# Expert rows loaded in four column strips and turned by VectorE instead of TensorE, with the expert weights stored to match

## The reference, cut to what matters

```python
logits = x @ w_gate                      # x: 4352 x 512
e_idx = np.argmax(logits, axis=1)
gate_w = probs[np.arange(N), e_idx]      # softmax of the logits
eom = 1.0 / (1.0 + np.exp(-(x @ w_output_gate)))
for e in range(E):                       # E = 8
    mask = e_idx == e
    h = np.maximum(x[mask] @ w1[e], 0.0) # w1[e]: 512 x 1024
    ye = h @ w2[e]                       # w2[e]: 1024 x 512
    out[mask] = gate_w[mask, None] * eom[mask, e, None] * ye
```

## Time and profile before

| | |
|---|---|
| median of three runs | 1226.95 us (1226.36 to 1226.95) |
| the profiled execution: its own time | 1227.15 us |
| the profiled execution: span of the trace | 1225.3 us |
| PE busy | 1189.3 us, 97% of the span |
| DVE busy | 580.4 us, 47% |
| ACT busy | 445.3 us, 36% |
| mean granted TensorE clock | 0.986 of full |
| row loads `xg<-buckets` | 41, 258.0 KB each, median 2.6 us from issue to landing |

### The profile page before, as it was taken

How to read it: one execution, slowest core, us unless ns; L and a number is a source line. 1 busy time by engine, 2 the same in 40 slices (tenths; PEclk the granted TensorE clock), 3 DMA queues, 4 the chain that set the end, 5 groups by cost and what they waited for, 6 DMA issues and landing times.

```text
span 1225.3 us, 20849 instructions
## 1 busy us (share of the span) xinstructions
PE 1189.3 (97%) x6808; PEld 939.2 (77%) x6809; DVE 580.4 (47%) x1100; ACT 445.3 (36%) x741; POOL 84.0 (7%) x96
## 2 busy tenths in 40 slices
PE   7999999999999999999999978999999999999995
PEld 6777777777777777777778866888888888878874
DVE  4564645645547455465554373553532223455221
ACT  3454434443444344443544332341411112344110
POOL 0000100101001000010010110200000000000000
PEclk8999999999999999999999988999999999999998
DMA  9110100001001111010100662514151110541111
GB/s 369 63 36 1 69 36 35 36 35 70 35 14 56 36 47 58 1 70 1 69 36 1 221 207 100 179 43 175 37 179 52 34 51 28 181 163 44 41 36 42
DMA packets 32266, 91.45 MB, mean 75 GB/s; under 512 B 2879, under 2 KB 4031, under 8 KB 29632
## 3 DMA queue, kind: packets, MB, share of 16 engines
q1 hardware_dynamic: 26432, 72.56, 17.0%
q0 software_dynamic: 5760, 17.90, 3.8%
HBM read 65.95 MB, written 25.55 MB: 75 GB/s over the span
## 4 chain that ended last, share of the span: by engine, by line
PE 93%; DVE 3%; ACT 1%; issue 1%; DMA 0%; DVEq 0%; ACTq 0%; POOL 0%; SPq 0%; POOLq 0%
PE y_ps L829 30%; PE h_ps L894 17%; PE y_ps L920 17%; PE h_ps L814 14%; PE y_ps L906 3%; PE a_ps L789 2%; PE h_ps L804 2%; PE a_ps L876 1%; PE a_ps L679 1%; PE a_ps L767 1%; PE a_ps L740 1%; PE b_ps L687 1%; DVE we L462 1%; PE b_ps L679 0%; DMA x_t<-in_x_t 0%
## 5 line engine op out<-in xcount | busy, mean ns | idle before, releaser
L829 PE MATMUL y_ps<-w_out_hi,hid_hi 128*128 128x512 f32 x544 | 220.4, 405 | 0.3 <-DVE w_out_lo L1328 0.3
L829 PE MATMUL y_ps<-w_out_hi,hid_lo 128*128 128x512 f32 x544 | 212.8, 391 | 0.0
L829 PE MATMUL y_ps<-w_out_lo,hid_hi 128*128 128x512 f32 x544 | 212.5, 391 | 0.0
L894 PE MATMUL h_ps<-we,xg_t_hi 128*128 (+1 forms) x608 | 195.5, 403 | 4.6 <-DVE we L462 2.0
L920 PE MATMUL y_ps<-we,act_t_hi 128*128 (+1 forms) x608 | 191.4, 396 | 2.2 <-issue 2.2
L814 PE MATMUL h_ps<-att_hi,mix 128*128 128x512 f32 x512 | 186.6, 408 | 0.0
L1343 DVE SCALAR_TENSOR_TENSOR hid<-hid,h_ps 128x512 f32<-128x512 f32 (+1 forms) x144 | 94.4, 655 | 182.8 <-ACT hid L1038 181.3
L1038 ACT ACTIVATE hid<-h_ps,three 128x512 f32<-128x512 f32 (+1 forms) x144 | 95.5, 663 | 204.2 <-PE h_ps L814 180.8
L829 PEld LDWEIGHTS y_ps<-w_out_hi,hid_hi 128*128 128x128 f32 x544 | 102.1, 188 | 51.2 <-issue 30.4
L894 PEld LDWEIGHTS h_ps<-we,xg_t_hi 128*128 128x128 f32 x608 | 112.2, 189 | 30.6 <-issue 6.2
L920 PEld LDWEIGHTS y_ps<-we,act_t_hi 128*128 128x128 f32 x608 | 111.4, 188 | 24.3 <-issue 2.7
(11 more groups left out here) (227 smaller groups left out, 1341.6 us busy)
## 6 DMA issues: line engine op xcount, KB each, us to landing
raw<-in_w SPq DMA_DIRECT2D x14, 2048.0 KB, 8.8
xg<-buckets SPq DMA_DIRECT2D x41, 258.0 KB, 2.6
xb<-in_x_rows SPq DMA_DIRECT2D x8, 1024.0 KB, 4.8
x_t<-in_x_t SPq DMA_DIRECT2D x7, 1024.0 KB, 5.5
buckets<-pad_row SPq DMA_DIRECT2D x8, 774.0 KB, 8.6
w_in_raw<-in_w_in SPq DMA_DIRECT2D x4, 1024.0 KB, 13.2
raw_out<-in_w_out SPq DMA_DIRECT2D x4, 1024.0 KB, 14.8
x_t_second<-in_x_t SPq DMA_DIRECT2D x1, 1024.0 KB, 19.7
```

The lines of the kernel that those rows point to most:

```text
L829: i = pe.matmul(y_ps[:, t, :], (hid_hi, hid_lo)[hp][:, hid_at(b, j), t * P:(t + 1) * P], w_out_s[wp][:, j, :], start=(j == 0 and m == 0), ...
L894: i = pe.matmul(hid_ps[:, h, :], xg_t[xp][:, slot % 2, k, :], we[:, bass.ds(w_at + (wp * WPART + k * F + h * BANK), BANK)], start=(k == 0 ...
```

## The change

A tile's rows are no longer loaded with one row on each partition. Column quarter j (128 columns) of all 128 rows goes to partitions 32j to 32j+31: partition 32j+t holds rows t, 32+t, 64+t and 96+t, 128 columns each. Four DMAs do this, and a fifth one loads the last four columns (gate factor and token number) of each row to a new tile `gate_s`. DVE then turns the tile by one `transpose`, which swaps partition and column within every 32x32 block, into `xg_raw`. `xg_raw` lies at the same address as `xg_t[LO]`; `rows_lo` subtracts in place. Partition 32j+d, chunk k of the result holds column 128j+32k+d, so w1 is stored in DRAM in that order of its rows, [E, 128, 4, F]; w2 is stored as [E, 128, 8, 512]. Both are then loaded with one contiguous run for each partition. PE's `transpose_rows` is gone.

```
@@ addresses
-    xg = at("xg", 163840, [P, RING, ROW], F32)
+    STRIPS = P // NS
+    xg = at("xg", 163840, [P, RING, STRIPS, P], F32)
+    gate_s = sb("gate_s", [P, RING, ROW - DM])
+    xg_raw = at("xg_raw", late_at + 12288, [P, 2, KD, P], F32)
@@ SP, load_rows
-            sp.dma_start(xg[:, slot, :], buckets[bass.ds(r, P), :]).then_inc(sem(f"xg_loaded{slot}"), 16)
+            tile_rows = buckets[bass.ds(r, P), :]
+            for j in range(STRIPS):
+                sp.dma_start(xg[NS * j:NS * j + NS, slot, :, :],
+                             tile_rows[:, P * j:P * j + P].rearrange("(s t) c -> t s c", t=NS)
+                             ).then_inc(sem(f"xg_loaded{slot}"), 16)
+            sp.dma_start(gate_s[:, slot, :], tile_rows[:, DM:ROW]).then_inc(sem(f"gate_loaded{slot}"), 16)
@@ SP, load_expert (the first loads likewise)
-            sp.dma_start(raw1[:].rearrange("p (k f) -> p k f", k=KD),
-                         w1[bass.ds(e, 1)].rearrange("o (k p) f -> p (o k) f", p=P)).then_inc(sem("raw1_loaded"), 16)
+            sp.dma_start(raw1[:], w1[bass.ds(e, 1)].rearrange("o p k f -> p (o k f)")
+                         ).then_inc(sem("raw1_loaded"), 16)
@@ PE
-        def transpose_rows(t):
-            slot = t.slot
-            wait(pe, f"xg_loaded{slot}", 16 * (t.turn() + 1))
-            wait(pe, "xg_t_ready", t.n)
-            for k in range(KD):
-                i = pe.transpose(a_ps[:, 0, k * P:(k + 1) * P], xg[:, slot, k * P:(k + 1) * P], ident[:])
-            i.then_inc(sem("xg_t_ps"), 1)
...
-            if not t.last:
-                transpose_rows(t.plus(1))
...
-        transpose_rows(Tile(0, 0))
@@ ACT, rows_hi
-            wait(act, "xg_t_ps", t.n + 1)
-            act.activation(xg_t[HI][:, slot % 2, :, :].rearrange("p k t -> p (k t)"), a_ps[:, 0, :], ACT.Copy
+            wait(act, "xg_turned", t.n + 1)
+            wait(act, "hid2_ps", HALVES * (t.n - 1) if not t.first else 0)
+            act.activation(xg_t[HI][:, slot % 2, :, :], xg_raw[:, slot % 2, :, :], ACT.Copy
@@ DVE, rows_lo subtracts from xg_raw in the place of a_ps; new beside it:
+        def turn_rows(t):
+            slot = t.slot
+            wait(dve, f"xg_loaded{slot}", 16 * STRIPS * (t.turn() + 1))
+            if not t.first and not is_b(t.n, 1):
+                wait(dve, "hid2_ps", HALVES * (t.n - 1))
+            dve.transpose(xg_raw[:, slot % 2, :, :].rearrange("p k t -> p (k t)"),
+                          xg[:, slot, :, :].rearrange("p s (k d) -> p k s d", d=NS)).then_inc(sem("xg_turned"), 1)
@@ DVE, start of the experts' part
         dve.tensor_copy(table[:, T_NEXT, MT:MT + 1], second[:]).then_inc(sem("second_ready"), 1)
+        turn_rows(Tile(0, 0))
         split_lo(dve, 1, 0, 0, (0,))
         rows_lo(Tile(0, 0))
...
         dve.sem_inc(sem("table_ready"), 1)
+        turn_rows(Tile(0, 1))
         split_lo(dve, 1, 0, 0, range(1, PIECES), "w2_ready")
@@ DVE, put_out waits for gate_loaded and reads gate_s; at the end of DVE's body(t):
+            if not (isinstance(t.n, int) and t.n + 2 >= MT):
+                turn_rows(t.plus(2))
```

More of the change, by code:

```diff
@@ L45, in emit_kernel @@
     E = w1.shape[0]
-    F = w1.shape[2]
+    F = w1.shape[3]
     SCALE = float(D) ** -0.5
@@ L524, in _ @@
         sp.wait_ge(sem("lt_ps"), B - 1)
-        sp.dma_start(raw1[:].rearrange("p (k f) -> p k f", k=KD),
-                     w1[0].rearrange("(k p) f -> p k f", p=P)).then_inc(sem("raw1_loaded"), 16)
+        sp.dma_start(raw1[:], w1[0].rearrange("p k f -> p (k f)")).then_inc(sem("raw1_loaded"), 16)
         sp.wait_ge(sem("pad_row_ready"), 2)
@@ L539, in _ @@
         sp.wait_ge(sem("h_ps"), KF * (B + 1))
-        sp.dma_start(raw2[:].rearrange("p (j d) -> p j d", j=KE), w2[0].rearrange("(j p) d -> p j d", p=P)
-                     ).then_inc(sem("raw2_loaded"), 16)
+        sp.dma_start(raw2[:], w2[0].rearrange("p j d -> p (j d)")).then_inc(sem("raw2_loaded"), 16)
         def load_rows(t):
@@ L555, in load_expert @@
             wait(sp, "w1_ready", n)
-            sp.dma_start(raw1[:].rearrange("p (k f) -> p k f", k=KD),
-                         w1[bass.ds(e, 1)].rearrange("o (k p) f -> p (o k) f", p=P)).then_inc(sem("raw1_loaded"), 16)
+            sp.dma_start(raw1[:], w1[bass.ds(e, 1)].rearrange("o p k f -> p (o k f)")
+                         ).then_inc(sem("raw1_loaded"), 16)
             wait(sp, "w2_ready", n)
-            sp.dma_start(raw2[:].rearrange("p (j d) -> p j d", j=KE),
-                         w2[bass.ds(e, 1)].rearrange("o (j p) d -> p (o j) d", p=P)).then_inc(sem("raw2_loaded"), 16)
+            sp.dma_start(raw2[:], w2[bass.ds(e, 1)].rearrange("o p j d -> p (o j d)")
+                         ).then_inc(sem("raw2_loaded"), 16)
         sp.wait_ge(sem("rows_stored"), 16 * N_SCATTER)
@@ L583, in all_loaded @@
                 tiles = min(t.n + RING, MT)
-                sp.wait_ge(sem(f"xg_loaded{s}"), 16 * ((tiles - s + RING - 1) // RING))
+                sp.wait_ge(sem(f"xg_loaded{s}"), 16 * STRIPS * ((tiles - s + RING - 1) // RING))
+                sp.wait_ge(sem(f"gate_loaded{s}"), 16 * ((tiles - s + RING - 1) // RING))
         loops(sp, body, all_loaded)
@@ L1397, in rows_lo @@
             wait(dve, "xg_t_hi", t.n + 1)
-            dve.tensor_tensor(xg_t[LO][:, slot % 2, :, :].rearrange("p k t -> p (k t)"), a_ps[:, 0, :],
-                              xg_t[HI][:, slot % 2, :, :].rearrange("p k t -> p (k t)").bitcast(F32), ALU.subtract
+            dve.tensor_tensor(xg_t[LO][:, slot % 2, :, :], xg_raw[:, slot % 2, :, :],
+                              xg_t[HI][:, slot % 2, :, :].bitcast(F32), ALU.subtract
                               ).then_inc(sem("xg_t_ready"), 1)
+        def turn_rows(t):
[5 more added lines that the diff above has]
+                          xg[:, slot, :, :].rearrange("p s (k d) -> p k s d", d=NS)).then_inc(sem("xg_turned"), 1)
         steps = [0]
@@ L1507, in put_out @@
                 wait(dve, f"out_stored{prev.slot}", 16 * (prev.turn() + 1))
-            dve.tensor_copy(out_row[:, slot:slot + 1], xg[:, slot, TOKEN:TOKEN + 1])
-            dve.tensor_scalar(yo[slot % 2][:], y2_ps[:, slot % 2, :], xg[:, slot, GATE:GATE + 1], None, ALU.mult
+            wait(dve, f"gate_loaded{slot}", 16 * (t.turn() + 1))
+            dve.tensor_copy(out_row[:, slot:slot + 1], gate_s[:, slot, TOKEN - DM:TOKEN - DM + 1])
+            dve.tensor_scalar(yo[slot % 2][:], y2_ps[:, slot % 2, :], gate_s[:, slot, 0:1], None, ALU.mult
                               ).then_inc(sem("out_ready"), 1)
@@ L1583 @@
     give("gates", gates.reshape(-1, 128, 4 * E).transpose(1, 0, 2))
-    give("w1", inputs["moe2_w1"])
-    give("w2", inputs["moe2_w2"])
+    give("w1", inputs["moe2_w1"].reshape(E, 4, 4, 32, -1).transpose(0, 1, 3, 2, 4).reshape(E, 128, 4, -1))
+    give("w2", inputs["moe2_w2"].reshape(E, -1, 128, DM).transpose(0, 2, 1, 3))
     n = B * (S + NS)
```

## The result

The changed kernel takes 1209.25 us (median of four runs, 1208.65 to 1210.2), the kernel before beside it 1226.65 us: a ratio of 0.986 with a 95% interval of 0.9843 to 0.9878, 17.4 us less. The profiled execution took 1208.73 us, with a span of 1207.0 us.

What follows compares the result with a forecast made beforehand. PE, busy 97% of the span, was taken to bound the steady tiles with its matmuls, DVE's chain the start; -16.3 + 2.3 - 0.9 = -14.9 us from 1227.15 gave 1212.3, as median 1212.0, range 1208.5 to 1218.5.

Steps and rivals of the forecast that it cites:

- PE's 0.44 us a tile: Steady tiles on PE: removing the four row transposes saves 0.44 us in each of 37 tiles, 16.3 us.
- the low bound of 0.35: Lower price of a tile's four row transposes on PE, from the spacing of their starts: 0.35 us, 13.0 us in all.
- the full duration of 272 ns: Rival for PE's row transposes: each saves its whole 272 ns, 40.3 us in all, giving 1188 us; chance 0.01.
- The junction: PE from `first` to `second`: its sequencer is over 2 us ahead, so closing the gap costs nothing.
- A turn of 0.7 us: DVE's transpose of a tile's rows takes 0.7 us, bounds 0.42 and 2.8, hidden in steady tiles.
- The start, 2.3 us: Start, on DVE's chain: a wait for strips and two turns, 0.9 + 0.7 + 0.7, delay the relu by 2.3 us.
- The term for the strips' wait: Start: DVE waits 0.9 us for tile 0's last strip, issued about 1.1 us after row 0's load, landing in 2.6.
- The stall, 0.9 us: Three-tile expert: PE's 1.98 us wait for w1's split shortens by about 0.9 us; bounds 0 and 1.98.
- The loads: SP's queue: five DMAs a tile for one, 0.33 us each; rows still arrive in time, so nothing is charged.
- The slower rival: Strips land too late for the four-tile loop; landing above 19.6 us takes back all gain; near 1250 us; chance 0.03.
- The sum: Whole kernel: the terms -16.3 + 2.3 - 0.9 give -14.9 us.

Runs made afterwards that it cites:

- e2: The changed kernel with four row transposes a tile put back on PE behind `first`, their result read by nobody: 1226.57 us.
- e3: The changed kernel with every tile turned twice by DVE, the second turn waiting for the first: 1211.58 us.
- e1: The kernel before with only the stored order of w1 and w2 and their loads changed: 1226.93 us, ratio 1.0001.
- e8: As e7, and ACT and DVE read their three table entries at the top of every body but the first: 1204.12 us.
- e5: The changed kernel with 155 small matmuls in the place of 100 before tile 0: 1210.38 us.
- e4: The changed kernel with each strip loaded by two DMAs of 64 columns in the place of one: 1213.23 us.
- e7: The changed kernel with 155 small matmuls for 100 and three pieces of w2's first split moved to the end of DVE's first body: 1206.97 us.
- e11: The changed kernel with the w2 split pieces moved, table entries read early and 130 small matmuls in the place of 100: 1205.43 us.

## Why the prediction was right, and where it was off

**PE's 0.44 us a tile.** Right: 0.46. The forecast took 37 * 0.44 = 16.3; measured are 36 * 0.46 = 16.6 and one more in tile 1, 17.0. The rest is in the w2 matmuls, whose piece on the chain is 5.47 us for 5.49. e2 settles the cause: the same 17.3 us come back when PE does idle transposes. It also settles that the low bound of 0.35 and the full duration of 272 ns were wrong prices.

**The junction.** Right: `second` follows `first` without a gap; the lead of PE's sequencer was enough. Only in the last tiles, behind the hardware loop, did some of the saved time come back, ahead of `first`: the chain has 0.19 and 0.17 us of issue there, for 0.09 and 0.09 before.

**A turn of 0.7 us.** Right: 701 ns, close to the 690 ns of the plain one-pass operation on 128x512 in the earlier trace rows. The Trainium skill (Vector Engine (DVE) Microarchitecture Reference, section 3.8) has the transposing front end sustain one element per cycle and lane; the trace agrees in that the turn takes as long as a plain pass over as many elements. The turn is hidden in the steady part even when doubled (e3).

**The start, 2.3 us.** The mechanism was right; the size was 1.5 in this profile. The term for the strips' wait was 0.9 and measured 0.39: SP took 0.44 us for a strip and not 0.33, but the data of the last strip was there 1.9 us after its issue and not 2.6. The two turns cost 0.64 us each on DVE's chain, and 0.3 us came back because the small operations around them ran that much earlier than before, counted from the last MLP matmuls. Counted so, DVE's relu moved by 1.35 us. e2, whose only edit is PE's idle transposes, has 2.2 us in the place of 1.5 because DVE came to its first turn 0.8 us later, and the kernel before with the weights' order changed (e1) starts 0.5 us later than before with no turn at all. So one profile each does not settle whether 2.3 was too much. The wait itself goes up to 2.30 us (e8) where a code load falls in with the strips, as told at e5.

**The stall, 0.9 us.** Nearly right: 0.74. ACT's split moved 2.35 us after its relu, as the step said, and DVE's was held by its relu and table reads; e8 shows that these reads are what was left of the stall.

**The loads.** The conclusion, nothing charged, was right; its number was not. The step took the longest landing before, 8.1 us, as the bound. Behind two weight loads the four strips took 12.6 us, and e4, with 14.4 and a later issue, shows PE 1.6 us late. The step was right that PE needs the turned rows only one tile later; what it did not work out is how little of that tile is left behind such a load, some 2.3 us. The slower rival asked for over 19.6 us in every tile; it overlooked that a single late tile, behind a weight load, already costs PE time.

**The sum.** 14.9 forecast, 17.4 measured. The terms as measured in the profiles, -17.0 + 1.5 - 0.7, give -16.2; the table without its first line gives -18.42 + 1.85 = -16.6, and the gap of 0.48 us that is gone is most of the rest. The difference between either and 17.4 is within what two medians of four runs are uncertain by (the interval of the ratio is 4.3 us wide). How much of it is the granted clock of tile 1's `first`, 7.24 us here and 8.5 in the profiles of e5, e7 and e8, is open. So the main term was hit closely and for its reason. The measured time lies near the fast end of the range, and of the 2.5 us by which the sum was short no more than about 1.7 can be traced to its terms.

## What to carry to other kernels

When one engine sets the pace, price what leaves it by the spacing of starts on the chain, not by durations, and check that its sequencer runs far enough ahead to close the gap. Moving work to an engine with half of its time free is free only where that engine does not lead: look separately at the start, where it often does. An in-order engine that waits for a DMA holds everything behind it, so the landing that counts is the longest one behind the largest transfer in the same queue. A change in the number of instructions on one engine can also move when code is loaded, so look at the DMA queues at that place before a difference is put down to the clock.

## What the runs showed of the hardware that was not expected

- Four strips of 64 KB, issued right behind two loads of 2 MB on SP, had landed 12.6 us after the first issue (the changed kernel); the same rows in eight DMAs took 14.4 us (e4). With no weight load ahead, the last strip was there 1.9 us after its issue.
- Issuing a strip on 32 partitions took SP about 0.44 us (1.76 for four), a whole-row load on 128 took 0.33.
- Where a code load of 0.02 MB fell among the strips of tile 0 (e5, e7, e8, e11), DVE waited 1.25 to 2.30 us for them, in the other six kernels with five loads 0.39 us or less. In e2, where it came at 728 to 730 us, SP needed 2.77 us to issue four strips at 729.28, for 1.81 in the changed kernel. That one causes the other is not shown.
- A fp32 transpose of 32x32 blocks over 128x512 took VectorE 701 ns (the changed kernel, median of 40).
- The granted clock of PE is not set by the program alone. Between 12 and 25 us, with the same instructions, its mean was 0.74 (before), 0.87 (e1) or 1.00 (after). Tile 1's `first` took from 5.86 to 8.56 us after PE had waited for other engines. What decides between the levels stays open.
